# Thresholds exchanged between two engines, key scaling moved, the second MLP's buffers rehoused and its first steps moved into the first MLP

## The reference

```python
# q, k, v: (4, 8, 576, 64); tau = 0.02
scores = matmul(q, k^T) / sqrt(64)
thresh = max(scores, -1) - tau
scores = where(scores >= thresh, scores, -1e9)
attn   = exp(scores - max(scores, -1))
x      = matmul(attn / (sum(attn) + 1e-9), v)        # -> (2304, 512)

h   = x @ w_in1                                      # (2304, 1024)
sm  = exp(h - max(h)) / (sum(exp(h - max(h))) + 1e-9)
s   = h * sm
ln  = (s - mean(s)) / sqrt(var(s) + 1e-6) * g_ln
y   = ln @ w_out1                                    # (2304, 512)

h2  = y @ w_in2                                      # (2304, 2048)
g   = max(h2, 0) + log1p(exp(-abs(h2)))
out = g @ w_out2                                     # (2304, 512)
```

## Time and profile before

| | before |
|---|---|
| median of 3 runs | 900.24 us (900.02 to 900.76) |
| profiled execution, its own time | 898.82 us |
| its span, first to last instruction | 897.1 us |
| TensorE's granted clock over the span | 0.998 |
| PE busy | 865.2 us (96%) |
| PE weight loads | 718.7 us (80%) |
| DVE busy | 634.2 us (71%) |
| ACT busy | 566.3 us (63%) |
| POOL busy | 331.4 us (37%) |

### The profile page before, as it was taken

How to read it: one execution, slowest core, us unless ns; L and a number is a source line. 1 busy time by engine, 2 the same in 40 slices (tenths; PEclk the granted TensorE clock), 3 DMA queues, 4 the chain that set the end, 5 groups by cost and what they waited for, 6 DMA issues and landing times.

```text
span 897.1 us, 16879 instructions
## 1 busy us (share of the span) xinstructions
PE 865.2 (96%) x6248; PEld 718.7 (80%) x6248; DVE 634.2 (71%) x1286; ACT 566.3 (63%) x1040; POOL 331.4 (37%) x425
## 2 busy tenths in 40 slices
PE   6799999999989999999999899999999999999998
PEld 4566666666667889898899798999899899899896
DVE  4999999999955633614431999767767767767765
ACT  2778898787866533424442876667667667667664
POOL 2555677555534601102110433323323323323322
PEclk9999999999999999999999999999999999999999
DMA  6623413343000100000001710000000000000000
GB/s 169 176 68 81 109 43 83 90 106 114 10 1 13 36 1 1 2 1 1 1 12 31 252 36 1 35 1 1 36 1 1 36 1 1 35 0 0 35 0 35
DMA packets 30394, 37.16 MB, mean 41 GB/s; under 512 B 4720, under 2 KB 18544, under 8 KB 30320
## 3 DMA queue, kind: packets, MB, share of 16 engines
q1 hardware_dynamic: 29920, 35.90, 14.3%
q10 hardware_dynamic: 400, 0.30, 0.1%
HBM read 31.46 MB, written 4.72 MB: 40 GB/s over the span
## 4 chain that ended last, share of the span: by engine, by line
PE 38%; issue 21%; POOL 10%; ACT 1%; DVE 1%; POOLq 0%; ACTq 0%
PE h_ps L943 12%; PE y_ps L1076 11%; POOL w_lo L487 10%; PE f_ps L1136 7%; PE m_ps L1052 6%; PE lt_ps L1088 1%; PE o_ps L1014 1%; ACT p_sb L551 0%; DVE ln_lo L809 0%; DVE g_lo L888 0%; ACT ln_hi L588 0%; POOLq L486 0%; DVE g_hi L886 0%; ACT u L679 0%; ACT w_hi L511 0%
## 5 line engine op out<-in xcount | busy, mean ns | idle before, releaser
L487 POOL TENSOR_TENSOR w_lo<-w_raw,w_hi 128x512 fp32r<-128x512 f32 x96 | 135.0, 1406 | 298.6 <-ACT w_hi L663 298.4
L540 ACT ACTIVATE expd<-s_ps,ntop 128x576 f32<-128x576 f32 x144 | 105.6, 741 | 55.4 <-DVE ntop L749 55.4
L663 ACT CAST w_hi<-w_raw 128x512 fp32r<-128x512 f32 x96 | 59.7, 622 | 119.2 <-PE f_ps L1136 118.2
L872 DVE SCALAR_TENSOR_TENSOR g<-u,z 128x384 f32<-128x384 f32 x96 | 63.3, 660 | 95.7 <-ACT u L679 95.7
L1052 PE MATMUL m_ps<-y_hi,w_lo 128*128 128x384 f32 x384 | 131.0, 341 | 0.0
L1052 PE MATMUL m_ps<-y_lo,w_hi 128*128 128x384 f32 x384 | 129.8, 338 | 0.0
L1052 PE MATMUL m_ps<-y_hi,w_hi 128*128 128x384 f32 x384 | 128.5, 335 | 0.0
L1136 PE MATMUL f_ps<-w_hi,g_hi 128*128 128x512 f32 x288 | 114.2, 396 | 4.0 <-DVE g_lo L888 3.2
L749 DVE TENSOR_REDUCE ntop<-s_ps 128x1 f32<-128x576 f32 x144 | 106.8, 757 | 14.1 <-PE s_ps L974 9.9
L765 DVE SCALAR_TENSOR_TENSOR kept<-s_ps,thresh,expd 128x576 f32<-128x576 f32 x144 | 112.1, 816 | 6.6 <-POOL thresh L426 3.5
L974 PE MATMUL s_ps<-k_sb,q_sb 64*128 64x288 f32 x512 | 96.5, 460 | 18.2 <-DVE kept L765 17.4
(11 more groups left out here) (88 smaller groups left out, 1744.9 us busy)
## 6 DMA issues: line engine op xcount, KB each, us to landing
q_sb<-q_t SPq DMA_DIRECT2D x28, 288.0 KB, 5.0
v_sb<-v_main SPq DMA_DIRECT2D x16, 256.0 KB, 3.2
stage<-w_in SPq DMA_DIRECT2D x16, 256.0 KB, 2.8
w_raw<-w_out SPq DMA_DIRECT2D x8, 512.0 KB, 5.6
out<-o_sb SPq DMA_DIRECT2D x5, 768.0 KB, 3.5
k_sb<-k_t SPq DMA_DIRECT2D x21, 144.0 KB, 4.6
stage<-w_in SPq DMA_DIRECT2D x4, 512.0 KB, 7.8
stage<-w_out SPq DMA_DIRECT2D x4, 512.0 KB, 6.5
```

What stands on the lines that cost most here:

```text
L487: nc.gpsimd.tensor_tensor(w4[1][:, n % 2, :], w4_raw[:, n % F2, :], f32(w4[0][:, n % 2, :]), ALU.subtract).then_inc(w4lo_made, 1)
L540: nc.scalar.activation(expd[:, tile % 2, :].rearrange("p (a b) -> p a b", a=2), s_ps[tile % 2][:, :, 0:HALF], ACT.Exp, bias=ntop[:, tile % ...
```

## The change

Four things are changed together.

1. In attention DVE makes the threshold of b and POOL that of a. POOL scales the second half of the first keys not at the start but after the third double. For the last but one group, POOL's work is split over two doubles and its sums are inverted earlier.
2. The end of attention: `hidden(0)` is placed in two halves behind two steps of attention, and the first half of `hidden(1)` behind a third. The two `x_low` of the first tiles are moved from the doubles 68 and 69 to behind DVE's last keep. ACT makes the exponential and the square of row tile 0 within attention's last steps.
3. Buffers: w3 is 16 tensors of their own, placed where the first MLP's buffers come free at different times; the first two pieces of w4 have a buffer of their own (`w4_first`).
4. The end of the first MLP: eight pieces of w3 are split into high and low before the first `soft`, 12 before the second MLP's own loop; four `up` stand before the last `project` (before, two and two behind it), and ACT and DVE do `soft` of blocks 0 to 3 beside that `project`. SP loads w4's first rows early and the other seven loads in one row after the last `project`.

```diff
-AHEAD = 4
-EARLY = 2
+EARLY = 4
+PREPARED = 12
...
+        w4_first = sb("w4_first", [P, 2, DM])
...
-        w3_lo = sb("w3_lo", [P, C, DFF2], FP32R, where=phase)
...
+        def w3_item(n):
+
+            w3_items[n] = sb(f"w3_{n}", [P, 2, C, P], FP32R, where=phase)
...
+            sp.wait_ge(y_made, C * MG)
+            for m in range(1, F2 // 2):
+                load_w4(m)
...
-            for image, loaded in enumerate((k_head, k_in)):
-                for pair in range(2):
...
+            for pair in range(2):
+                scale_first_keys(pair, 0)
+
+            def make_threshold_a(u):
+
+                pool.wait_ge(top_made, 2 * u + 1)
+                col = slice(2 * u % 4, 2 * u % 4 + 1)
                 nc.gpsimd.tensor_scalar(thresh[:, col], ntop[:, col], -1.0, tau_sb[:, 0:1], ALU.mult, ALU.subtract
-                                        ).then_inc(thresh_b, 1)
...
+                                        ).then_inc(thresh_a, 1)
...
             for u in range(DOUBLES + 1):
                 if u < DOUBLES:
-                    make_threshold_b(u)
+                    make_threshold_a(u)
+                if u == DOUBLES - 1:
+                    probabilities(GROUPS - 2, [2])
                 for group in complete(u - 1):
-                    probabilities(group)
+                    if group != GROUPS - 2:
+                        probabilities(group)
+                if u == DOUBLES - 2:
+                    probabilities(GROUPS - 2, [0, 1])
+                if u == 2:
+                    for pair in range(2):
+                        scale_first_keys(pair, 1)
...
                     maximum(b)
-                    make_threshold_a(u)
+                    make_threshold_b(u)
...
-                if u in (68, 69):
-                    x_low(0, u - 68)
+                    if group == GROUPS - 2:
+                        invert(group)
+            for n in range(2):
+                x_low(0, n)
...
-                if v == DOUBLES:
+                if DOUBLES <= v < DOUBLES + 2:
 
                     pe.wait_ge(kept_made, TILES)
                     pe.wait_ge(xlo_made, 1)
-                    hidden(0, 0)
-            pe.wait_ge(xlo_made, 2)
-            hidden(1, 1)
+                    hidden(0, 0, (v - DOUBLES,))
+                if v == DOUBLES + 2:
+                    pe.wait_ge(xlo_made, 2)
+                    hidden(1, 1, (0,))
+            hidden(1, 1, (1,))
...
-                    j = tile - (MT - 2)
-                    if j == 1:
+                    if tile == MT - 2:
+                        first_up(0)
+                        first_up(1)
+                    else:
 
                         pe.wait_ge(ltlo_made, MT - 2)
                         transpose_row(tile, n % 2)
-                    first_up(j)
+
+                        pe.wait_ge(ltlo_made, MT - 1)
+                        first_up(2)
+                        first_up(3)
```

More of the change, by code:

```diff
@@ L147, in build @@
         names = "top ntop esum esum_e inv ssum nmean sq msq var rstd"
-        st = {n: sb("st_" + n, [P, 2], where=phase) for n in names.split()}
-        first_words = 2 * 2 * C * P + 6 * DFF1 + 2 * len(st)
+        st_all = sb("st", [P, 32], where=phase)
+        st = {n: st_all[:, 2 * k:2 * k + 2] for k, n in enumerate(names.split())}
+        first_words = 2 * 2 * C * P + 6 * DFF1 + 32
         sb("gap1", [P, SCORE_WORDS - first_words], where=phase)
@@ L551, in transposed, with row_exponential, row_square @@
                 nc.scalar.copy(out, t_ps[q][:, :].rearrange("p (x k c) -> p x k c", x=2, k=KT)).then_inc(p_made, 1)
+            def row_exponential(i, n):
+                tile, slot = 6 * i + n, n % 2
+                col = slice(slot, slot + 1)
+                act.wait_ge(hntop_made, tile + 1)
+                nc.scalar.activation(e1[:, slot, :], h_ps[slot][:, :], ACT.Exp, bias=st["ntop"][:, col],
+                                     accum_out=st["esum"][:, col]).then_inc(e1_made, 1)
+            def row_square(i, n):
+                tile, slot = 6 * i + n, n % 2
+                col = slice(slot, slot + 1)
+                act.wait_ge(mean_made, tile + 1)
+                wait(act, msq_made, tile - 1)
+                nc.scalar.activation(e1[:, slot, :], solu[:, slot, :], ACT.Square, bias=st["nmean"][:, col],
+                                     accum_out=st["sq"][:, col]).then_inc(sq_made, 1)
             for v in range(DOUBLES + LAG_T // 2 + LAG_V):
@@ L692, in soft, with first_w3, next_w3 @@
                 logarithm(j, n)
-            for j in range(F2):
-                if j + AHEAD < F2:
-                    w_high(C + F1 // 2 + j + AHEAD)
+            def first_w3(m):
+                if m == 0:
+                    act.wait_ge(h_made, MT)
+                    for n in range(3):
+                        w_high(W3 + n)
+                if m == 1:
+                    y_high(0, 0)
+                    w_high(W3 + 3)
+                if m == 2:
+                    for n in range(4, 7):
+                        w_high(W3 + n)
+            def next_w3(m):
+                if m == 0:
+                    w_high(W3 + 9)
+                    soft(3, 3)
+                if m == 1:
+                    w_high(W3 + 10)
+                if m == 2:
+                    act.wait_ge(lt_made, MT - 1)
+                    w_high(W3 + 11)
+            for n in range(6):
+                mlp1(0, n)
+                if n >= 2:
+                    if n == 2:
+                        act.wait_ge(o_made, SIXES)
+                        act.wait_ge(x_made, SIXES)
+                    w_high(C + n - 2)
+            with act.Fori(1, MT // 6) as i:
+                for n in range(6):
+                    mlp1(i, n)
+            for n in range(3):
+                mlp1(MT // 6, n)
+            w_high(W3 + 7)
+            act.wait_ge(ones_made, 6)
+            act.wait_ge(ln_made, MT)
+            soft(0, 0)
+            mlp1(MT // 6, 3)
+            soft(1, 1)
+            w4_high(0, 0)
+            w4_high(1, 1)
+            w_high(W3 + 8)
+            soft(2, 2)
+            mlp1(MT // 6, 4)
+            w4_high(2, 2)
+            w4_high(3, 3)
+            for j in range(EARLY, F2):
+                if j - EARLY + PREPARED < F2:
+                    w_high(W3 + j - EARLY + PREPARED)
                 soft(j, j)
-                m = j // 2
-                act.wait_ge(w4_in[m % W4_LOADS], 16 * (m // W4_LOADS + 1))
                 w4_high(j, j)
@@ L857, in mlp1 @@
                 if isinstance(i, int) and tile == MT - 1:
-                    for m in range(EARLY):
+                    for m in range(7):
+                        if m == 3:
+                            y_low(0, 0)
                         w3_low(m)
-                    y_low(0, 0)
                 if after_product(i, n):
                     transposed_low(i, n - 2)
+                if isinstance(i, int) and tile == MT:
+                    w3_low(7)
             three_parts(dve, MT + 4, 6, mlp1, MT // 6)
@@ L903, in outputs @@
                     nc.vector.tensor_copy(o_sb[:, k, :], f_ps[k][:, :]).then_inc(f_out, 1)
-            for m in range(EARLY, AHEAD):
-                w3_low(m)
             def mlp2(i, n):
@@ L934, in _, with hidden @@
             pe.wait_ge(zero_made, 4)
-            def hidden(tile, slot):
-                for a in range(DFF1 // BANK):
+            def hidden(tile, slot, sides=(0, 1)):
+                for a in sides:
                     for k in range(C):
```

162 lines of the change are left out of this document (84 added, 78 removed).

## The result

| | before | after |
|---|---|---|
| median | 900.13 us (899.59 to 900.76, 4 runs) | 887.94 us (886.36 to 888.86, 4 runs) |
| ratio | | 0.9863, 95% interval 0.9848 to 0.9877 |
| profiled execution | 898.82 us, span 897.1 | 887.9 us, span 886.2 |
| PE busy | 865.2 us | 861.7 us |
| DVE, ACT, POOL busy | 634.2, 566.3, 331.4 us | 638.6, 567.1, 324.3 us |

The account below looks back on a forecast made before the run. PE's work or waits bound the kernel, with DVE's chain holding two of three doubles in attention. Gains of 3.9 + 3.7 + 0.7 + 0.9 + 3.8 = 13.0 us gave 885.8 profiled, median 887.2 us, range 884 to 892.

Parts of the forecast that it names:

- Start of attention: First doubles of attention: DVE keeps b directly behind a, without waiting for POOL; net gain 3.9 us, bounds 2.5 and 4.3.
- The exchange in the other doubles: Attention's loop: keep of a freed of its wait, three doubles from 10.18 to about 10.00; gain 3.7 us.
- The rival that the loop does not move: Attention's loop stays as it is because the exponential or PE holds it; 890.9 us, chance 0.17.
- `x_lo`: Two doubles late in attention lose their x_lo, which moves behind the last keep and is hidden; gain 0.67 us.
- end of attention: Behind the last scores, PE's waits of 0.30 and 0.83 go, less two more changes of product kind; gain 0.9 us.
- the wait that stays: Behind the last scores, PE's wait of 1.18 us, ended by ACT's copy of the left-over columns, stays.
- Start of the second MLP: PE's waits of 0.65, 2.72 and 0.46 go; gain 3.8 us, bounds 2.5 and 4.1.
- The 1.4 between the median and the profiled execution: Whole kernel: the median lies 1.4 us above the profiled execution, so 885.8 gives 887.2 us.
- a granted clock of 0.89: Doubles 1 to 2 of attention: clock lowered after PE idled some 3.6 us; its end gains 0.2 us.
- Blocked thresholds: DVE's threshold waits for POOL's long steps in eleven doubles; loss 8.2 us, 895.4 us, chance 0.05.

Follow-up runs that it names:

- e1_layout: Kernel before, with only w3's placing changed: each of its two tensors keeps its 16 pieces one behind the other; 899.98 us, ratio 1.0001.
- g3_before_aligned: Kernel before, with every large array at a multiple of 64 bytes and nothing else changed; 897.25 us, ratio 0.9972.
- g4_pairs: Kernel before, with each item of w3 holding its high and low part side by side; 898.18 us, ratio 0.9978.
- e2_scaling: Kernel before, with only POOL's scaling of the first keys' second halves moved behind the third double; 894.86 us, ratio 0.9949.
- e3_exchange: Kernel before, with only the thresholds exchanged (POOL makes a's, DVE b's); 902.42 us, ratio 1.0027.
- f3_clock: Changed kernel, with six more idle transpositions on PE in each of doubles 3, 4 and 5; 886.52 us, ratio to before 0.9854.
- f4_soft_late: Changed kernel, with ACT's four first `soft` behind the last `project` as before; 905.21 us, ratio to the kernel before 1.0053.
- g2_aligned: Changed kernel with both thresholds on POOL, idle transpositions in doubles 3 to 5, one multiplication ahead, large arrays at multiples of 64 bytes; 879.59 us.
- f1_thresholds_back: Changed kernel, with only the thresholds given back (a on DVE, b on POOL); 885.76 us, ratio to the kernel before 0.9844.

## Why the prediction was right, and where it was not

- **Start of attention:** right, and a little small (4.5 against 3.9). Of the 0.6 more, 0.4 is that the first keep came at 8.80 and not at 9.19; it comes at 8.84, 8.86 and 8.84 in e1_layout, g3_before_aligned and g4_pairs too, which leave the start as it was, so this is chance and no work of the change. The cost of the moved scalings is there: doubles 2 to 3 took 3.56 (15.64, 19.20) against 3.40, since the fourth keep waits behind them. e2_scaling shows that the part brings this alone.
- **The exchange in the other doubles:** this is the step that failed, "freed of the semaphore it could start at 0.09" and "I take 3.7". I had freed the keep of its producer and not counted that the threshold now standing ahead of it had got a producer just ahead of itself. The rival that the loop does not move was the true one for this term (chance 0.17, 890.9), and its reason was not the one that I gave it: neither the exponential nor PE held the loop, since with both thresholds off DVE it went to 9.92 at once.
- **`x_lo`, end of attention, the wait that stays:** right to 0.1 us.
- **Start of the second MLP:** right in kind, small in size: 5.0 against 3.8. The listed waits make 3.83. Of the rest, 1.2, one half lies in blocks that were longer before by more than their listed waits: the first two (4.46 and 4.30, after 4.18 and 4.17), the one with the wait of 0.46 (4.81) and the one behind it (4.30). The other half lies ahead of the first `down`, in small gaps that I did not list; I have not split it further.
- **Pace of the second MLP:** not in the prediction at all, 1.8. g4_pairs shows that w3's placing does it. Together with the start's surplus and that of the second MLP (0.6, 1.2 and 1.8) it filled the hole of 3.8 that the exchange left, all but the 1.9 lost in doubles 5 to 7. None of this had been foreseen: that the sum of the profiled execution is only 2.1 off is luck.
- **The 1.4 between the median and the profiled execution:** taken over from before, and wrong after the change (0.04). By e1_layout's trace it was the price of a longer and of a second fall of the clock, behind two waits that the change ended. This made up for 1.4 of the 2.1.
- **The clock's fall in double 6:** not foreseen. The prediction named a granted clock of 0.89 in attention's start before and took its end for a gain; the idle of 3.58 ended and its fall of the clock with it, but shorter idles in doubles 3 to 5, which had been harmless at 1.45, 1.20 and 1.35, became 1.63, 1.14 and 1.80, and three of four executions have a mean clock below 1.000.
- **Blocked thresholds:** this rival did not come true. DVE's threshold beside POOL's two-input work, in the kernel after:

```profile
105.66 2.51 POOL L442 TENSOR_TENSOR w_lo<-stage,w_hi 128x512 fp32r<-128x512 f32 x2
...
106.06 0.21 DVE L843 TENSOR_SCALAR thresh<-ntop,tau_sb 128x1 f32<-128x1 f32 x1
```

It takes its usual 0.21 in the midst of it. Eleven thresholds run beside the subtraction or the keys' scaling, as counted in the prediction, and all 72 take 0.212 to 0.217. The Trainium skill, "SBUF — State Buffer", section "Who interferes with whom", would have the two shut each other out if this step ran in a two-port mode; the trace shows no such thing for one element per partition.

Open: what the 0.34 us of "issue" in double 5 is. It belongs to the exchange: it stands at the same keep in the four kernels in which DVE makes the threshold of b (the kernel after, e3_exchange, f3_clock, f4_soft_late) and in none of the other ten. A second one, at the keep of a in double 63, is 0.36 in the seven kernels in which DVE makes a's threshold, 0.26 in those four, and absent in the three in which POOL makes both. Open too is which property of an address makes `up` and `down` faster.

## What to carry to other kernels

When work is exchanged between engines to free an instruction of its neighbour, look at what comes to stand in the freed place and how old its inputs are: a small step behind its own producer costs as much as the one it replaced, and only taking it off the engine helps. Where a loop's start is made faster, look again at every short idle of PE behind it, since here the clock fell behind three idles of which two had grown, by 0.2 and 0.45 us. And when buffers are rehoused, compare the pace of a stretch in which PE never waits: an unchanged loop may run 0.5% faster or slower by its addresses alone, which can hide or feign the effect under study.

## What the runs showed of the hardware

- The pace of the same matmuls depends on where their operands lie in on-chip memory: with PE without a gap, a block of 12 products of 384 columns and 9 of 512 takes 4.200, 4.180 or 4.173 us in six placings (4.200: before, e1_layout; 4.180: after, g4_pairs, g2_aligned; 4.173: g3_before_aligned).
- A 128x1 step on DVE starts 0.79 behind the start of the 0.75 us reduction whose result it reads, and a step with other inputs 0.68 behind one of 0.76: the dependence costs about 0.1 us. Before, where the reduction just ahead was not the one it read, the same step started 0.67 behind it.
- In the kernel after the granted clock fell in the midst of the work, at 0.74, 0.50 and 0.90 in the stretches 28 to 30, 30 to 32 and 32 to 34 us, after PE had waited 1.63, 1.14 and 1.80 us ahead of three scores; waits of 1.45, 1.20 and 1.35 in the same doubles (kernel before, f1_thresholds_back) left it at 1.00, and six transpositions more in each of three doubles kept it at 1.00. Values that took 1.52 us at 2.4 GHz took 2.83 then.
